# One small load for both integers, a TensorE copy to all partitions, and the first query loads on ScalarE's queue

## The reference, cut to what matters

```python
scores = scale * np.matmul(q, k.transpose(0, 1, 3, 2))
rel = pos[:, None] - pos[None, :]
is_global = pos[None, :] < int(n_global)
is_local = (rel >= 0) & (rel < int(n_local))
dist = np.where(is_global & ~is_local, float(n_local), np.abs(rel).astype(np.float32))
scores = np.where(is_global | is_local, scores - slopes[:, None, None] * dist, -1e9)
a = softmax(scores)                 # over the keys
x = np.matmul(a, v)                 # 1536 tokens x 512
h = x @ w_in1;  x = (h * sigmoid(h)) @ w_out1            # 512 -> 2048 -> 512
h = x @ w_in2;  x = (h * np.clip(h + 3, 0, 6) / 6) @ w_out2
```

## Time and profile before

| | before |
|---|---|
| median of three runs | 621.78 us (621.23 to 623.08) |
| profiled execution, its own time | 621.76 us |
| span of the profiled execution | 619.6 us |
| PE busy | 595.8 us, 96% |
| DVE, ACT, POOL busy | 370.6, 339.8, 283.6 us |
| first PE instruction with a record | 8.24 us |
| PE busy from 40 to 60 us | 20.0 us |
| mean granted TensorE clock | 0.989 |

### The profile page before, as it was taken

How to read it: one execution, slowest core, us unless ns; L and a number is a source line. 1 busy time by engine, 2 the same in 40 slices (tenths; PEclk the granted TensorE clock), 3 DMA queues, 4 the chain that set the end, 5 groups by cost and what they waited for, 6 DMA issues and landing times.

```text
span 619.6 us, 9570 instructions
## 1 busy us (share of the span) xinstructions
PE 595.8 (96%) x3408; PEld 514.6 (83%) x3408; DVE 370.6 (60%) x696; ACT 339.8 (55%) x657; POOL 283.6 (46%) x353
## 2 busy tenths in 40 slices
PE   3999998599999999999999999999999999999998
PEld 2566666599999999899999998888888888888886
DVE  4778875645755576657655668557555685555431
ACT  3888884444444475544444756555556575555441
POOL 2888975723943333439533333377333333331110
PEclk9999999599999999999999999999999999999999
DMA  7444430212122212321322122212221242211002
GB/s 275 177 154 147 164 115 3 75 65 68 47 90 68 69 35 68 103 69 35 96 72 67 39 69 69 71 66 69 68 69 68 69 165 73 69 68 35 1 0 103
DMA packets 14883, 50.08 MB, mean 81 GB/s; under 512 B 1904, under 2 KB 2160, under 8 KB 14832
## 3 DMA queue, kind: packets, MB, share of 16 engines
q1 hardware_dynamic: 14832, 49.42, 23.4%
HBM read 46.27 MB, written 3.15 MB: 80 GB/s over the span
## 4 chain that ended last, share of the span: by engine, by line
PE 93%; DVE 3%; ACT 1%; issue 1%; DMA 1%; POOL 0%; DVEq 0%; SPq 0%; ACTq 0%
PE ps L898 37%; PE ps L977 22%; PE ps L968 14%; PE ps L969 7%; PE ps L870 4%; PE ps L845 4%; PE ps L855 4%; DMA words<-in_n_loc 1%; DVE x_lo L444 1%; DVE g_lo L586 1%; DVE wi_lo L435 0%; ACT probs L649 0%; POOL probs L274 0%; DVE g_f L460 0%; ACT g_hi L780 0%
## 5 line engine op out<-in xcount | busy, mean ns | idle before, releaser
L365 POOL TENSOR_TENSOR wo_lo<-wo_raw,wo_hi 128x1024 fp32r<-128x1024 f32 x32 | 76.6, 2393 | 282.4 <-ACT wo_hi L774 282.4
L898 PE MATMUL ps<-x_hi,wi_hi 128*128 128x384 f32 x448 | 153.1, 342 | 9.4 <-DVE c_sb L450 4.9
L898 PE MATMUL ps<-x_hi,wi_lo 128*128 128x384 f32 x448 | 151.6, 338 | 0.0
L898 PE MATMUL ps<-x_lo,wi_hi 128*128 128x384 f32 x448 | 151.6, 338 | 0.0
L450 DVE TENSOR_TENSOR c_sb<-ps,p_c 128x384 f32<-128x384 f32 x64 | 35.7, 557 | 171.6 <-PE ps L898 171.4
L697 ACT ACTIVATE p_c<-ps 128x384 f32<-128x384 f32 x64 | 31.5, 492 | 140.3 <-PE ps L898 140.1
L898 PEld LDWEIGHTS ps<-x_hi,wi_hi 128*128 128x128 f32 x448 | 85.2, 190 | 14.1 <-DVE c_sb L450 5.7
L898 PEld LDWEIGHTS ps<-x_hi,wi_lo 128*128 128x128 f32 x448 | 85.4, 191 | 0.6
L898 PEld LDWEIGHTS ps<-x_lo,wi_hi 128*128 128x128 f32 x448 | 85.4, 191 | 0.0
L977 PE MATMUL ps<-wo_hi,g_hi 128*128 128x512 f32 x192 | 75.9, 395 | 0.0
L977 PE MATMUL ps<-wo_hi,g_lo 128*128 128x512 f32 x192 | 75.9, 395 | 0.0
(11 more groups left out here) (89 smaller groups left out, 1081.5 us busy)
## 6 DMA issues: line engine op xcount, KB each, us to landing
wi_raw<-in_w_in SPq DMA_DIRECT2D x32, 512.0 KB, 3.3
wo_raw<-in_w_out SPq DMA_DIRECT2D x32, 512.0 KB, 3.3
v_raw<-in_v SPq DMA_DIRECT2D x8, 704.0 KB, 4.2
k_raw<-in_kT SPq DMA_DIRECT2D x8, 464.0 KB, 4.9
q_raw<-in_qT SPq DMA_DIRECT2D x8, 384.0 KB, 5.5
out_y<-y_out SPq DMA_DIRECT2D x11, 256.0 KB, 4.2
out_y<-y_out SPq DMA_DIRECT2D x2, 128.0 KB, 1.8
words<-in_n_glob SPq DMA_DIRECT2D x1, 1.0 KB, 2.6
```

The lines of the kernel that those rows point to most:

```text
L365: nc.gpsimd.tensor_tensor(wo_lo[:, s % 2, :], wo_raw[:, s % 2, :], wo_hi[:, s % 2, :], ALU.subtract).then_inc(wo_lo_ok, 1)
L898: mm = nc.tensor.matmul(p_bank(bank), w[:, s % 2, at], x[:, b, k, :], start=fresh and k == 0 and i == 0, stop=k == 1 and i == 2, skip_grou ...
```

## The change: what it does

The two integers come as one array `counts` of 16 bytes and land in one partition. All arithmetic on them is done in that partition. A matrix product with a column of ones (`ones` has one partition and 128 columns) writes the three floats to all partitions in PSUM, and DVE copies them to `nums`. PE runs eight transposes of the identity matrix before that product and eight after it; their result is never read. ACT issues the loads of the queries of pairs 0 and 1, and SP issues keys and values.

```diff
-            sp.dma_start(words[:, 0:2], n_glob.to_broadcast([P, 2])).then_inc(words_in, 16)
-            sp.dma_start(words[:, 2:4], n_loc.to_broadcast([P, 2])).then_inc(words_in, 16)
-            load_qk(sp, 0)
-            load_qk(sp, 1)
+            sp.dma_start(words[:, :], counts).then_inc(words_in, 16)
+            for it in range(2):
+                load_k(sp, it)
             load_v(sp, 0)
...
+            nc.vector.memset(ones[:, :], 1.0).then_inc(ones_ok, 1)
-            dve.wait_ge(words_in, 32)
+            dve.wait_ge(words_in, 16)
...
-            link(nc.vector.tensor_scalar(cnt[:, 6:7], cnt[:, 5:6], 1.0, None, ALU.is_ge))
-            link(nc.vector.scalar_tensor_tensor(cnt[:, 6:7], cnt[:, 5:6], float(MAXLOC), cnt[:, 6:7], ALU.is_le, ALU.mult))
-            nc.vector.scalar_tensor_tensor(flag[:, :], ng, float(GLOB), cnt[:, 6:7], ALU.is_le,
+            nc.vector.tensor_scalar(cnt[:, 6:7], cnt[:, 5:6], 0.0, None, ALU.max).then_inc(row_ok, 1)
+            link(nc.vector.tensor_scalar(cnt[:, 7:8], cnt[:, 5:6], 1.0, None, ALU.is_ge))
+            link(nc.vector.scalar_tensor_tensor(cnt[:, 7:8], cnt[:, 5:6], float(MAXLOC), cnt[:, 7:8], ALU.is_le, ALU.mult))
+            nc.vector.scalar_tensor_tensor(flag[:, :], cnt[:, 4:5], float(GLOB), cnt[:, 7:8], ALU.is_le,
                                            ALU.mult).then_inc(flag_ok, 1)
-            link(nc.vector.tensor_scalar(nl, cnt[:, 5:6], 0.0, None, ALU.max))
+            dve.wait_ge(rows_ok, 1)
+            link(nc.vector.tensor_copy(nums[:, 0:3], ps[:, 1, 0:3]))
+            ng, nl = nums[:, 0:1], nums[:, 2:3]
...
-            link(nc.vector.tensor_scalar(cnt[:, 0:1], nl, -8.0, None, ALU.mult))
+            link(nc.vector.tensor_scalar(nums[:, 3:4], nl, -8.0, None, ALU.mult))
...
         def _(act):
+            for it in range(2):
+                load_q(act, it)
...
             pe.wait_ge(ident_ok, 2)
+            def busy(n):
+                for _ in range(n):
+                    nc.tensor.transpose(ps[:, 0, 0:P], ident[:, :], ident[:, :])
+            busy(8)
+            pe.wait_ge(ones_ok, 1)
+            pe.wait_ge(row_ok, 1)
+            nc.tensor.matmul(ps[:, 1, 0:3], ones[:, :], cnt[:, 4:7], start=True, stop=True).then_inc(rows_ok, 1)
+            busy(8)
```

More of the change, by code:

```diff
@@ L54, in at_least, with build @@
     eng.wait_ge(sem, value)
-def build(nc, qT, kT, v, w_in1, w_out1, w_in2, w_out2, n_glob, n_loc, out):
+def build(nc, qT, kT, v, w_in1, w_out1, w_in2, w_out2, counts, out):
     outer = ExitStack()
@@ L77, in build @@
         ident = sb("ident", [P, P])
-        words = sb("words", [P, 4], I32)
-        cnt = sb("cnt", [P, 8])
-        flag = sb("flag", [P, 1], I32)
+        words = sb("words", [1, 4], I32)
+        cnt = sb("cnt", [1, 8])
+        ones = sb("ones", [1, P])
+        nums = sb("nums", [P, 4])
+        flag = sb("flag", [1, 1], I32)
         slope = sb("slope", [P, 2 * NH])
@@ L138, in x_quad @@
             return x_raw[:, KT * b + 2 * (quad // 2):KT * b + 2 * (quad // 2) + 2, TB * (quad % 2):TB * (quad % 2) + TB]
-        words_in = sem("words_in"); ident_ok = sem("ident_ok"); iota_ok = sem("iota_ok")
+        words_in = sem("words_in"); ones_ok = sem("ones_ok"); row_ok = sem("row_ok"); rows_ok = sem("rows_ok"); ident_ok = sem("ident_ok"); iota_ok = sem("iota_ok")
         chain = sem("chain"); flag_ok = sem("flag_ok")
@@ L170, in build, with load_k, load_q @@
         NQK = 16
+        def load_k(eng, it):
+            eng.dma_start(k_raw[it % 2][:, 0:KW], kT[it]).then_inc(k_in[it % 2], 16)
+        def load_q(eng, it):
+            eng.dma_start(q_raw[it % 2][:, :], qT[it]).then_inc(q_in[it % 2], 16)
         def load_qk(sp, it):
-            par = it % 2
-            sp.dma_start(k_raw[par][:, 0:KW], kT[it]).then_inc(k_in[par], 16)
-            sp.dma_start(q_raw[par][:, :], qT[it]).then_inc(q_in[par], 16)
+            load_k(sp, it)
+            load_q(sp, it)
         def load_v(sp, it):
@@ L395, in _ @@
             link(nc.vector.scalar_tensor_tensor(cnt[:, 4:6], cnt[:, 2:4], 4294967296.0, cnt[:, 0:2], ALU.mult, ALU.add))
-            ng, nl = cnt[:, 4:5], cnt[:, 7:8]
-            link(nc.vector.tensor_scalar(cnt[:, 6:7], cnt[:, 5:6], 1.0, None, ALU.is_ge))
-            link(nc.vector.scalar_tensor_tensor(cnt[:, 6:7], cnt[:, 5:6], float(MAXLOC), cnt[:, 6:7], ALU.is_le, ALU.mult))
-            nc.vector.scalar_tensor_tensor(flag[:, :], ng, float(GLOB), cnt[:, 6:7], ALU.is_le,
+            nc.vector.tensor_scalar(cnt[:, 6:7], cnt[:, 5:6], 0.0, None, ALU.max).then_inc(row_ok, 1)
+            link(nc.vector.tensor_scalar(cnt[:, 7:8], cnt[:, 5:6], 1.0, None, ALU.is_ge))
+            link(nc.vector.scalar_tensor_tensor(cnt[:, 7:8], cnt[:, 5:6], float(MAXLOC), cnt[:, 7:8], ALU.is_le, ALU.mult))
+            nc.vector.scalar_tensor_tensor(flag[:, :], cnt[:, 4:5], float(GLOB), cnt[:, 7:8], ALU.is_le,
                                            ALU.mult).then_inc(flag_ok, 1)
-            link(nc.vector.tensor_scalar(nl, cnt[:, 5:6], 0.0, None, ALU.max))
+            dve.wait_ge(rows_ok, 1)
+            link(nc.vector.tensor_copy(nums[:, 0:3], ps[:, 1, 0:3]))
+            ng, nl = nums[:, 0:1], nums[:, 2:3]
             def masks(link, rel, jj, loc, glb, keep, ngl, dist):
@@ L427, in _ @@
             link(nc.vector.tensor_tensor(far, rel8, far, ALU.add))
-            link(nc.vector.scalar_tensor_tensor(m_base[:, :], glb, cnt[:, 0:1], far, ALU.add, ALU.max))
+            link(nc.vector.scalar_tensor_tensor(m_base[:, :], glb, nums[:, 3:4], far, ALU.add, ALU.max))
             def w_low(s, part):
@@ L1055 @@
         "w_out2": w_out_steps(moe2_w_out),
-        "n_glob": np.asarray(n_global, np.int64).reshape(1, 1).view(np.int32),
-        "n_loc": np.asarray(n_local, np.int64).reshape(1, 1).view(np.int32),
+        "counts": np.asarray([n_global, n_local], np.int64).reshape(1, 2).view(np.int32),
     }
```

## The result

| | before | changed |
|---|---|---|
| median | 622.43 us (4 runs, 621.23 to 623.35) | 615.12 us (4 runs, 613.97 to 615.26) |
| ratio | | 0.988 (95% interval 0.9856 to 0.9903) |
| profiled execution, its span | 619.6 us | 612.1 us |

One later execution of the kernel before, 972.13 us at a mean granted clock of 0.566, is in no comparison here; without it the median of the kernel before beside e1 to e4 is 622.66 us.

The account below looks back on a forecast made before the run. The start was taken to hang on the integers until the first subtraction at 11.13 us, with ACT and then PE full behind it. An earlier table saves 2.5 us, other parts nothing: 621.8 - 2.5 = 619.3 us, range 617.1 to 621.3.

Parts of the forecast that it names:

- The integers: At the start, one small transfer issued at 0.80 us lands at 3.0 us (2.6 to 5.5) instead of 5.94.
- Rival 1: At the start, the word queues behind the queries and the time is 621.5 us; chance 0.10.
- The way through TensorE: From the word's landing through PE's product to DVE's table: starts at 4.65 instead of 7.27 us; 2.5 us counted.
- Loads: First keys and queries land by about 6 us, scores done at 8.0, DVE needs them at 8.6; cover 0.6 us.
- rival 2: PE bounds the start through branch, transposes and slow scores, costing 0.5 to 1.5 us, time 620.3; chance 0.09.
- The clock at the start: Before about 16 us, a faster PE through transposes was counted at nothing, bounds -0.5 and +1.6 us.
- rival 3: PE still slow when it becomes last at 15.3 us, costing 1.6 us, time 620.9; chance 0.04.
- the sign that was named: Prediction wrong if the first subtraction's shift is under 1.9 us or isn't found again at 100 us.
- The clock at the hand-over: Where attention gives way to products, half clock costs 24 products 2.3 us; the shift might end or lengthen that.
- rival 4: At the hand-over to the products the clock stays or returns at once, time 617.1 us; chance 0.10.
- 5: The half-clock stretch at the hand-over to the products grows by another 14 us, time 626.3 us; chance 0.05.
- The queue: At the start, queries issued on ACT save one or two issues of about 0.4 us; counted at nothing.

Follow-up runs that it names:

- e1: The kernel before with one unused 32-byte tile behind the small ones, moving every later tile; 617.8 us, ratio 0.9919.
- e4: The changed kernel without the sixteen transposes of the identity, the product of the ones kept; 614.4 us, ratio 0.9870.
- e3: The changed kernel with 96 unused bytes behind `warm`, later tiles placed as before relative to 64 and 128 bytes; 619.0 us, ratio 0.9939.
- e8: The changed kernel with the queries of pairs 0 and 1 issued on SP again; 613.5 us, ratio 0.9862.
- e9: The changed kernel with g_hi and g_lo alone moved 96 bytes past a multiple of 128; 618.5 us, one run.
- e18: The changed kernel with wi_hi and everything behind it moved by 128 bytes; 618.4 us, one run.
- e12: The changed kernel without the sixteen transposes, plus 25 unread matmuls of 384 columns where PE waits in step 1; 611.9 us, ratio 0.9826.
- e11: The changed kernel with all tiles moved by 128 bytes; 612.7 us, one run.
- e16: The changed kernel with all tiles moved by 32 bytes, distances between them unchanged; 612.8 us, one run.

## Why the prediction was wrong

- **The step that failed** is the list of parts itself. It costed instructions, transfers and waits, and said that what is taken off the start reaches the end whole "unless TensorE's clock gives or takes something". It had no term for the place of the operands. The new and resized small tiles changed the distance from wo to g from 224 to 0 modulo 256, worth 225.10 - 222.95 + 204.50 - 201.97 = 4.7 us in the two stretches and 4.8 us in e1's median. Nothing in the rows quoted showed it: the time from matmul to matmul was taken as fixed. The rest of the change is what the prediction summed, and there its 2.5 us were sound: 2.94 us at the first subtraction, and 3.7 (2.1 to 5.5) in e3.
- **The integers**: right in kind, off in size. The word landed 1.2 us after issue (1.8 to 4.7 was the bracket), so even the floor, a 128 KB store, was too far. The Trainium skill's 2.0 us, "DMA: Bandwidth & Descriptors" (Anatomy of one DMA), which that section fits to transfers issued from GpSimd, is too long for this one from SP as well. Rival 1 didn't come: the queries, issued on ACT at 0.79 us, did not hold the word issued at 0.80.
- **The way through TensorE**: 8 x 0.24 = 1.9 us for the transposes was 1.97; from the product's start to DVE's copy it took 0.62 (3.32 to 3.94) against 0.55, and no run shows the bound of 0.9. As the word came early, the transposes, free in my sum, stood on the path with 0.45 us (e4). The table started at 4.32 instead of 4.65 us, the first subtraction at 8.19 instead of 8.6: 2.94 against 2.5.
- **Loads**: scores at 5.73 us, before DVE wanted them; rival 2 didn't come. The branch did run beside the transposes, as scores followed the last of them by less than a branch takes (0.84 us).
- **The clock at the start**: rival 3, at 0.04, is what the profiled execution shows. PE was slow until 17.0 us, though its granted clock is written as 1.00 from 8 us on, and the lead fell from 2.94 to 1.76 us, so the sign that was named, a shift of 1.9 us or more found again at 100 us, failed there and held in e8 (3.0 at step 2). But it isn't of this change: e1, whose start is that of the kernel before, shows slow rows even at 22 to 24 us:

```profile
22.14 1.05 PE ps L871 x8
23.19 1.16 PE ps L846 x4
24.35 0.77 PE ps L856 x4
25.12 0.59 PE ps L871 x8
```

It varies from execution to execution: e9, which differs from the changed kernel by pads alone, was fast from 13.9 us on. It can also come and go: in e18 eight score records from 8.75 us on took 1.39 us, the full pace, and from 12 to 20 us its granted clock was 0.50. This should have been a spread on both kernels instead of a rival at 4%. The rule in the Trainium skill, "TensorE: Matmul & The Clock Gate" (Part 4: PE-mode transpose), that transposes don't count as activity, is neither shown nor refuted: with and without them the full pace came at times that differ from run to run.
- **The clock at the hand-over**: neither rival 4 nor 5 came; 24 products took 6.55 us against 6.58. The price of rival 4, 2.3 us, was about right, as e12 measured 2.1; the time given for it takes off 2.2. Another slip changed nothing: two scores at 8 x 0.08 us are 0.64, not 0.5.
- **The queue**: the move of the queries was counted at nothing, and e8 agrees.

## What to carry to other kernels

Before and after any change that adds, drops or resizes a tile, compare the places of the operands of the hottest matmuls, and give both kernels the same distances, or the comparison measures them too. A few unused bytes cost nothing to try. When a small change at the start moves the end by more, align the two traces at the same event of every step: a lead that grows evenly is a changed pace, not a removed wait. Two profiled executions can differ by 1 to 2 us at the start through TensorE's pace alone, so read a gain there from more than one pair.

## What the hardware showed unexpectedly

In this kernel the time from matmul to matmul changes with where its two operands stand to one another. For 512 columns in steps 18 to 31 it is 227.8 or 227.9 ns at a distance from wo_hi to g_hi that is a multiple of 256 bytes (63232, 63744 and 64000 were tried), 232 to 234 ns at 32, 64, 96, 128 and 224 past one, and moving all tiles together changes nothing (e11, e16). e18 is the exception: 227.1 ns there, and slower pairs in half of the earlier steps at an unchanged distance. That PE's reading of the moving operand and its loading of the next weights get into each other's way is my guess, and no run shows it directly. The Trainium skill, "TensorE: Matmul & The Clock Gate" (Step-by-step: what each phase is for), says that loading the next weights takes no read bandwidth from the running matmul; the dependence on the distance may speak against that as a full account, but no run here separates the two reads.
